# Attention and MLP interleaved on one core: value products in two lots over neighbouring steps, results turned and written one step later

## The reference

```python
scores = q @ k.T / 8                                   # 4 batches, 8 heads, 576 rows, 64 columns
scores = where(scores >= max(scores) - tau, scores, -1e9)
attn = exp(scores - max(scores)); attn /= sum(attn) + 1e-9
x = heads_side_by_side(attn @ v)                       # (4, 576, 512)
u = x + (x.T @ U @ V).T                                # token mixing, rank 32
x = u + relu(u @ w_ch1) @ w_ch2                        # 512 -> 2048 -> 512
logits, local_gate = x @ w_gate, sigmoid(x @ w_local)
# each row takes its own best expert, or keeps the one of the row before when local_gate >= 0.5
out[row] = p[e] * (relu(x[row] @ w1[e]) @ w2[e])       # 8 experts, 512 -> 1024 -> 512
```

## Time and profile before

| | us |
|---|---|
| median of 3 runs | 1241.75 (1239.94 to 1247.33) |
| the profiled execution, whole | 1242.59 |
| its span, first to last instruction | 1240.8 |
| steps 36 to 143 in it | 136.6 to 741.4 |

### The profile page before, as it was taken

How to read it: one execution, slowest core, us unless ns; L and a number is a source line. 1 busy time by engine, 2 the same in 40 slices (tenths; PEclk the granted TensorE clock), 3 DMA queues, 4 the chain that set the end, 5 groups by cost and what they waited for, 6 DMA issues and landing times. The chain is left out here.

```text
span 1240.8 us, 20479 instructions
## 1 busy us (share of the span) xinstructions
PE 1087.9 (88%) x7134; PEld 952.1 (77%) x7135; DVE 605.5 (49%) x1160; ACT 441.7 (36%) x727; POOL 367.9 (30%) x307
## 2 busy tenths in 40 slices
PE   3688799999989999999999898999516999999996
PEld 2555579898979989977989886999405777777775
DVE  1365555566455565645555642222493345243551
ACT  2355444333354333434433233111412244143541
POOL 2354104335410452430433430442171111111111
PEclk9999999999999999989999899999756999999999
DMA  6666404254361542443524212220442254143520
GB/s 151 150 165 154 96 1 125 63 130 115 79 163 30 130 121 82 117 129 67 125 62 113 68 35 72 65 73 1 174 135 94 94 176 168 51 151 118 178 97 34
DMA packets 111422, 128.82 MB, mean 104 GB/s; under 512 B 67373, under 2 KB 67373, under 8 KB 111344
## 3 DMA queue, kind: packets, MB, share of 16 engines
q1 hardware_dynamic: 106160, 116.15, 33.7%
q0 software_dynamic: 3520, 10.75, 2.7%
q10 hardware_dynamic: 1664, 0.89, 0.3%
HBM read 87.90 MB, written 10.22 MB: 79 GB/s over the span
## 5 line engine op out<-in xcount | busy, mean ns | idle before, releaser
L757 ACT ACTIVATE ex<-score_banks,stat 128x576 f32<-128x576 f32 x131 | 97.1, 741 | 208.4 <-DVE stat L855 208.4
L659 PE MATMUL mlp_banks<-hid_hi,w_hi 128*128 128x320 f32 (+1 forms) x512 | 158.1, 309 | 8.5 <-DVE z L922 7.3
L651 PE MATMUL mlp_banks<-u_hi,w_hi 128*128 128x320 f32 (+1 forms) x512 | 158.1, 309 | 8.2 <-DVE hid_lo L914 5.3
L482 POOL TENSOR_TENSOR w_lo<-stage,w_hi 128x1024 fp32r<-128x1024 f32 x64 | 152.9, 2389 | 4.6
L651 PE MATMUL mlp_banks<-u_hi,w_lo 128*128 128x320 f32 (+1 forms) x512 | 152.3, 297 | 0.0
L651 PE MATMUL mlp_banks<-u_lo,w_hi 128*128 128x320 f32 (+1 forms) x512 | 152.2, 297 | 0.0
L659 PE MATMUL mlp_banks<-hid_hi,w_lo 128*128 128x320 f32 (+1 forms) x512 | 151.8, 297 | 0.0
L659 PE MATMUL mlp_banks<-hid_lo,w_hi 128*128 128x320 f32 (+1 forms) x512 | 151.8, 296 | 0.0
L478 POOL CAST w_hi<-stage 128x1024 fp32r<-128x1024 f32 x64 | 66.6, 1041 | 268.8 <-PE mlp_banks L651 229.5
L865 DVE SCALAR_TENSOR_TENSOR ex<-score_banks,stat,ex 128x576 f32<-128x576 f32 x131 | 107.0, 816 | 61.3 <-ACT ex L757 50.0
L586 PE MATMUL score_banks<-k_tiles,q_tiles 128*128 128x288 f32 x580 | 106.3, 311 | 28.4 <-ACT et_first L767 12.3
(11 more groups left out here) (225 smaller groups left out, 2057.3 us busy)
## 6 DMA issues: line engine op xcount, KB each, us to landing
stage<-in_moe_w_ch SPq DMA_DIRECT2D x64, 512.0 KB, 3.9
w_raw<-in_moe_w SPq DMA_DIRECT2D x64, 512.0 KB, 4.8
q_tiles<-q_parts SPq DMA_DIRECT2D x32, 320.0 KB, 3.9
q_tiles<-q_parts SPq DMA_DIRECT2D x64, 160.0 KB, 4.2
k_tiles<-k_parts SPq DMA_DIRECT2D x60, 144.0 KB, 3.5
raw_q<-in_q SPq DMA_DIRECT2D x32, 128.0 KB, 2.6
raw_v<-in_v SPq DMA_DIRECT2D x32, 128.0 KB, 2.8
raw_k<-in_k SPq DMA_DIRECT2D x30, 128.0 KB, 2.7
```

Source lines behind the costliest of these rows:

```text
L482: nc.gpsimd.tensor_tensor(w_lo[:, n % RING], stage[:, n % 2], w_hi[:, n % RING].bitcast(F32), ALU.subtract).then_inc(w_split, 1)
L651: last = nc.tensor.matmul(bank[:, 0:w], ch1(a, g, d, c), of[:, d, cols], start=(d == 0 and n == 0), stop=(d == KC - 1 and n == 2))
L659: last = nc.tensor.matmul(bank[:, 0:w], ch2(a, g, q, c), of[:, q, 0:w], start=(q == 0 and n == 0), stop=(q == QUARTER - 1 and n == 2))
L757: nc.scalar.activation(ex_of(n), score_of(n), ACT.Exp, bias=stat[:, n % 4, 0:1], scale=-1.0).then_inc(exp_done, 1)
```

## The change

From the second batch on, half 1's value products stand in j = 0 (chunks 0 to 2) and j = 1 (chunks 3 and 4), half 0's in j = 4 and j = 5. `copy_out`, `turn_out`, `inverse` and `write_x` follow one step later. The plan of tasks moves along: token mixing goes from the third step of a batch to the fourth, and what is left over goes into the batch's last step, which takes three tasks in place of one. With the plan move the tasks that free weight slots, and with them POOL's and SP's places for the pieces (`SPLIT_AT`). One step more is counted behind the last block.

```diff
--- before.py
+++ after.py
@@ -102,10 +102,10 @@
             plan.append([])
             continue
         ready = NTASK * b - (TAIL if at < ALONE else 0)
-        if at < 2:
+        if at < 3:
             ready = NTASK * (b - 1)
             want = 4 if at == 0 else TAIL
-        elif at == 2:
+        elif at == 3:
             want = 1
         else:
             want = 3 if j in (6, 8) else 2
@@ -122,7 +122,7 @@
 
 
 FILL = tasks_by_step()
-NSTEP = max(len(FILL), NBLK + 2)
+NSTEP = max(len(FILL), NBLK + 3)
 FILL += [[]] * (NSTEP - len(FILL))
 STEP_OF = {t: n for n, ts in enumerate(FILL) for t in ts}
 
@@ -690,7 +690,6 @@
                 if j == 7:
                     values(p, 0, (3, 4))
             issue(s + 3) if s + 3 < LEAD + 2 else None
-        every = tuple(range(NT))
         for n in range(ALONE, NSTEP):
             p, j, _, _ = place(n)
             fill = FILL[n]
@@ -698,16 +697,20 @@
                 pe.wait_ge(et_copied, n)
                 scores(n + 1)
             if j == 0 and p <= PAIRS:
-                values(p - 1, 1, every)
+                values(p - 1, 1, (0, 1, 2))
             if p == PAIRS_OF and j == 1:
                 turn_out(p - 1, 0)
             if j == 1 and p <= PAIRS:
+                values(p - 1, 1, (3, 4))
+            if j == 2 and p <= PAIRS:
                 turn_out(p - 1, 1)
             if LED <= p + 1 < PAIRS and j < 3:
                 turn_part(p + 1, j)
             if j == 4 and p < PAIRS:
-                values(p, 0, every)
+                values(p, 0, (0, 1, 2))
             if j == 5 and p < PAIRS:
+                values(p, 0, (3, 4))
+            if j == 6 and p < PAIRS:
                 turn_out(p, 0)
             for t in fill[:1]:
                 task(t)
@@ -829,11 +832,11 @@
                 task(t)
             if n < NBLK:
                 copy_turned(n)
-            if j == 0 and p <= PAIRS:
+            if j == 1 and p <= PAIRS:
                 copy_out(p - 1, 1)
             if LED <= p + 1 < PAIRS and j < 3:
                 copy_part(p + 1, j)
-            if j == 4 and p < PAIRS:
+            if j == 5 and p < PAIRS:
                 copy_out(p, 0)
             for t in fill[1:]:
                 task(t)
@@ -967,11 +970,11 @@
                 mask(n + 1)
             if p == PAIRS_OF and j == 1:
                 write_x(p - 1, 0)
-            if j == 1 and p <= PAIRS:
+            if j == 2 and p <= PAIRS:
                 if p > PAIRS_OF:
                     inverse(p - 1, 4, 2 * NT)
                 write_x(p - 1, 1)
-            if j == 5 and p < PAIRS:
+            if j == 6 and p < PAIRS:
                 inverse(p, 0, 4)
                 write_x(p, 0)
             for t in fill:
```

## The result

The changed kernel takes 1276.5 us in the median (1273.74 to 1278.35, four runs), beside 1243.55 for the kernel before on the same chip: a ratio of 1.0263, 95% interval 1.0224 to 1.0302. That is 33 us slower. The forecast was +10.8 us, so its direction was right and its size wrong; the time lies outside the range as well. The profiled execution took 1277.22 us, its span is 1275.4 and its mean granted clock 0.951 (0.957 before).

The account below looks back on a forecast made before the run. TensorE was taken as the bound nearly everywhere, with about 29 us of waits in the interleaved stretch. The terms 6.0 + 0.6 + 0 + 2.1 + 3.0 - 0.9 gave +10.8 us, a median of 1252 us, range 1240 to 1262.

Parts of the forecast that it names:

- TensorE is the bound and the steady stalls keep their distance: Interleaved stretch: added matmuls cost full time; z stalls of steps 56, 92, 128 stay, 0.2 us longer each, +0.6 us.
- the "0" of the forecast: Stalls on hid_lo in steps 65 and 137: 5.3 us before, about 5.5 after, taken as 0; bounds -5.3 and +4.
- The lots' ends, +6.0: Value products: 25 halves split into two lots, 0.24 us each, +6.0 us; bounds 0 and 8.8.
- Steps with three tasks, +2.1: Steps with j = 6: x's first half on DVE delays tasks, 0.5 us in step 51, 0.2 in step 60; three batches.
- Rival (b): First half's inverse is caught by POOL's subtraction in step 51, held 2.3 us in three batches: 1259.4 us; chance 0.2.
- A batch's start, +1.0 each: Steps 71 to 79: idle 6.0 to 6.5 us against 4.6 to 4.9; +1.0 per batch, +3.0 in all.
- The end, -0.9: Behind step 143: the 0.9 us wait for the last copy goes; row copies and stores cover x's chain in step 146.
- The clock, 0: TensorE's lower-clock dips behind stalls fall by chance: +-4 us on any execution, zero in the sum.
- (a): Lock of DVE and POOL is missed; all five stalls and two clock dips go: 1235 us; chance 0.08.
- (c): Cheap splits and a neutral batch start: lot ends hide, step 74 costs no more, +3.7: 1245.5 us; chance 0.22.

Follow-up runs that it names:

- The two parts by themselves: Kernel before with only the new task plan, 1247.57 us; changed kernel with the old task plan (lots and later turn), 1255.89 us.
- the split alone: Kernel before with each half's value products in two lots within the same step, nothing else changed: 1249.84 us, ratio 1.0045.
- whole lots: Changed kernel with each half's value products in one lot again: 1286.94 us; the same with inversion first, five row buffers and early loads: 1237.94 us.
- all cures: Changed kernel with the inversion at the head of DVE's step, five row buffers, and batch-start weight loads ahead of row stores: 1239.39 us, ratio 0.9972.
- five buffers: Changed kernel with five buffers for row results instead of two: 1264.88 us, ratio 1.0152.
- early loads: Changed kernel with weight loads ahead of the row stores in a batch's first step only: 1265.88 us, ratio 1.0163.
- these two: Changed kernel with both five row buffers and weight loads ahead of row stores in a batch's first step: 1262.91 us, ratio 1.0160.
- the inversion first: Changed kernel with the inversion at the head of DVE's step: 1250.04 us, ratio 1.0066; the same move in the kernel before: 1228.71 us, ratio 0.9886.
- the cured kernel before: Kernel before with the inversion at the head of DVE's step and five row buffers: 1227.56 us, ratio 0.9886.

## Why the prediction was wrong, step by step

- **TensorE is the bound and the steady stalls keep their distance.** Right. The stalls on z stand in steps 57, 93 and 129 with 2.86 us, +0.4 each where +0.2 was said; those in steps 66 and 138 are 1.53 and 3.63 (before 1.70 and 3.63): the "0" of the forecast. The two parts by themselves show that the kept distance is the reason: when only one side moves, the stalls on z are gone.
- **The lots' ends, +6.0.** Right for the split alone: 5.6 by the run that does nothing else. In the changed kernel it isn't that price: whole lots gain 3.0 us with all cures (between -1 and +7) and lose 11 without.
- **Steps with three tasks, +2.1.** Half of its size. In steps 51, 87 and 123 PE is idle 1.67 us, where it was 0.23, 0.14 and 0.82: +3.8, and 0.25 in each of steps 60, 96 and 132, together the upper bound of 4.5. The step-51 sum held only x's 0.75 us on DVE. Unseen was that POOL's start moves too, against the threshold addition. It is held longer, in the kernel after:

```profile
215.98 2.39 POOL L482 TENSOR_TENSOR w_lo<-stage,w_hi 128x1024 fp32r<-128x1024 f32 x1
216.09 2.30 DVE L862 TENSOR_TENSOR stat<-stat,tau 128x1 f32<-128x1 f32 x1
...
219.23 0.17 DVE L885 TENSOR_SCALAR inv<-sums 128x4 f32<-128x4 f32 x1
219.44 2.37 POOL L482 TENSOR_TENSOR w_lo<-stage,w_hi 128x1024 fp32r<-128x1024 f32 x1
```

  Rival (b) had the inversion caught in this step. It escaped by 0.2 us.
- **A batch's start, +1.0 each.** This is the step that failed. In steps 36 to 43 idle time went from 6.95 to 7.00 us, less than forecast; in steps 72 to 79 from 3.8 to 9.8 and in 108 to 115 from 3.8 to 9.3. With the 4.5 us that the two mixings take longer at the lower clock, the +3.0 of the forecast measured about 16. The first batch has no rows to store. The step was worked out from the queues of ACT and DVE alone. I wrote that the weight splits follow the tasks, and used it for steps 63 to 66, but did not carry it to steps 70 to 73, where the loads pass behind the row stores. SP's queue was not read there at all. Nor did I ask what DVE's inversion would meet behind step 74 when the pieces come late. Beyond the waits, the longer idle time was followed by the lower clock under the mixing, 2.06 us in step 75.
- **The end, -0.9.** The same error. The 0.9 us before the products did go. But the "two row copies and the stores before them" were taken as cover; they are what is late. The last mixing waits 2.98 us in place of 0.86, and the tail is 5.6 us longer.
- **The clock, 0.** On the profiled execution the batches are 23.6 us longer, of which 14.6 is idle and 5.6 is lots' ends. The mixings at the lower clock (2.06 us in step 75, 2.43 in step 111, where it takes 6.99) are more than the 3.4 left, and other stretches at 1.2 GHz fall differently in the two executions. Under the mixing it looks like no chance: in the four kernels that cured the idle time or the wait for x only in part (five buffers, early loads, these two, the inversion first) the granted clock under that mixing was still 0.54 to 0.74, with all cures it was 1. That is one execution of each.
- **The rivals.** (a), a lock that is missed, names the right mechanism: moving the inversion out of POOL's way is worth 14 us before and about 25 after. The change as a whole doesn't do it, but each of its parts alone does. (b) and (c) did not occur. None had SP in it.

**The account by runs.** Of the 33 us, the lock and the late store with what hangs on them hold 22: the cures take 36 us from the kernel after (1.0263 to 0.9972) and 14 from the one before (1 to 0.9886; there the loads stand ahead of the stores as it is). The remaining 10.7 is what the change costs without them. What it is made of isn't shown term by term. The lots' ends are one part, and steps 51, 87 and 123 still wait 1.24 us each (0.06 or less in the cured kernel before), but elsewhere waits got shorter, and idle time in the three batches is only 1.2 us more (21.3 against 20.1). That the rest is the forecast's sum to a tenth is luck: its interval is 4 us either way, and its terms are not those of the forecast one by one.

**What stays open.** How the 36 us divide between the two mechanisms stays open. Taken alone they are worth 12.8 and 24.5 us by the ratios, 37 in sum, which is 36 within the intervals; but the inversion first also frees x from the late pieces, so this isn't a clean division. And whole lots in the cured kernel gain between -1 and +7 us; the intervals don't say more. What the lower clock under the mixing costs by itself wasn't tested apart from the waits.

## What to carry to other kernels

When a change shifts a plan by a step, list for every queue, the one that only issues transfers too, which instruction it issues in which step before and after, and look for pairs whose order changes. A transfer that passes in front of another can be paid by an engine that neither of them feeds. A short operation on SBUF tiles is better put ahead of the other engine's long one in the program's order than left to meet it: here that was worth 14 us of 1243 by itself. And the costs of the parts, measured alone, need not add up: here each part moved one side of a collision between two engines and so escaped it, while both together kept it. Run the whole and the parts, and compare their idle time stretch by stretch before the difference is given to one place.

## What the runs showed of the hardware

- A 256 KB store issued behind 1 MB of weight loads and 0.3 MB of v released its buffer 4.6 us after its issue; with only v ahead of it, 2.2. The Trainium skill (DMA: Bandwidth & Descriptors, Queues, rings and completion order) says that each DMA engine takes a queue's descriptors in ring order, so the store would wait for what was issued ahead of it; these two numbers agree.
- A one-column addition was held 2.30 us (kernel after, 216.09) and a six-column scaling 2.29 us by POOL's subtraction, each to its end. A reciprocal of six columns was not: in the kernel after with both cures it began at 245.02, inside a subtraction that ran from 244.85 to 247.25, and took 0.19 us.
- Ten mixing matmuls took 4.53 us at the upper level of the clock and 6.62 where those up to 368.1 ran at the lower (0.51), behind 4.26 and 2.36 us of idle time. Behind 1.17 and 1.44 us (five buffers and early loads) the clock was still 0.74 over that stretch, behind 1.19 and 0.19 (both cures) it was 1.00.
